# Routing of a mixture-of-experts layer in three batches, with token lists in DRAM and one expert tile ahead of the table

## The reference

```python
# 1: windowed attention with sinks -> x (3072, 512)
# 2: dense stage
h = x @ w_in                      # 512 -> 2048
x = (h * np.cos(h)) @ w_out       # 2048 -> 512
# 3: top-1 mixture of 8 experts
logits = x @ w_gate + modality_bias[modality_id]
e_idx = np.argmax(logits, axis=1)
probs = softmax(logits);  gate_w = probs[np.arange(N), e_idx]
for e in range(8):
    mask = e_idx == e
    h = np.maximum(x[mask] @ w1[e], 0.0)          # 512 -> 1024
    out[mask] = gate_w[mask, None] * (h @ w2[e])  # 1024 -> 512
```

## Time and profile before

| | us |
|---|---|
| median of 3 runs | 1177.29 (1176.71 to 1179.24) |
| profiled execution, its time | 1176.95 |
| profiled execution, its span | 1175.1 |
| PE busy in the span | 1118.3 (95%) |
| DVE busy | 720.3 (61%) |
| ACT busy | 482.8 (41%) |
| POOL busy | 87.6 (7%) |

### The profile page before, as it was taken

How to read it: one execution, slowest core, us unless ns; L and a number is a source line. 1 busy time by engine, 2 the same in 40 slices (tenths; PEclk the granted TensorE clock), 3 DMA queues, 4 the chain that set the end, 5 groups by cost and what they waited for, 6 DMA issues and landing times.

```text
span 1175.1 us, 20461 instructions
## 1 busy us (share of the span) xinstructions
PE 1118.3 (95%) x6348; PEld 935.4 (80%) x6349; DVE 720.3 (61%) x1849; ACT 482.8 (41%) x1079; POOL 87.6 (7%) x174
## 2 busy tenths in 40 slices
PE   6999999989999999999999999996799999999996
PEld 5777777767888888888888888885689999899895
DVE  7889888865458757757757757766663222342221
ACT  5777777754333333333333334332452211331221
POOL 0000000010000000000000000000121221221121
PEclk9999999999999999999999999997699999999998
DMA  5554544432002001002002000002672110131110
GB/s 121 147 146 145 145 132 135 138 116 87 1 1 72 1 1 71 0 0 72 0 0 72 0 0 36 1 1 106 202 235 68 54 54 19 40 120 38 36 53 17
DMA packets 34140, 78.72 MB, mean 67 GB/s; under 512 B 10414, under 2 KB 10414, under 8 KB 33968
## 3 DMA queue, kind: packets, MB, share of 16 engines
q1 hardware_dynamic: 29456, 65.60, 17.9%
q0 software_dynamic: 4640, 12.59, 3.2%
HBM read 60.87 MB, written 19.92 MB: 69 GB/s over the span
## 4 chain that ended last, share of the span: by engine, by line
PE 86%; DMA 3%; DVE 3%; SPq 3%; issue 3%; ACT 1%; POOL 0%; DVEq 0%; POOLq 0%; ACTq 0%
PE bank L1359 23%; PE bank L1373 23%; PE bank L1478 14%; PE bank L1466 12%; PE bank L1234 5%; DMA v_sink<-v_n 3%; PE bank L1268 3%; PE bank L1279 2%; PE bank L1246 2%; PE bank L1448 1%; SPq L405 1%; SPq L397 1%; PE bank L1439 1%; PE bank L1236 1%; SPq L400 0%
## 5 line engine op out<-in xcount | busy, mean ns | idle before, releaser
L1359 PE MATMUL bank<-x_hi,w_hi 128*128 128x512 f32 x384 | 152.4, 397 | 4.8 <-issue 4.1
L1194 DVE SCALAR_TENSOR_TENSOR h_lo<-bank,h_hi 128x256 fp32r<-128x256 f32 x112 | 47.5, 424 | 173.6 <-ACT h_hi L756 173.3
L1373 PE MATMUL bank<-w_hi,g_hi 128*128 128x512 f32 x384 | 152.3, 397 | 0.5 <-DVE g_lo L1009 0.5
L1359 PE MATMUL bank<-x_hi,w_lo 128*128 128x512 f32 x384 | 152.7, 398 | 0.0
L1359 PE MATMUL bank<-x_lo,w_hi 128*128 128x512 f32 x384 | 152.6, 397 | 0.0
L1373 PE MATMUL bank<-w_hi,g_lo 128*128 128x512 f32 x384 | 152.0, 396 | 0.0
L1373 PE MATMUL bank<-w_lo,g_hi 128*128 128x512 f32 x384 | 151.8, 395 | 0.0
L1478 PE MATMUL bank<-xg_hi,w_hi 128*128 128x256 f32 x448 | 127.4, 284 | 4.3 <-DVE xg_lo L1188 2.7
L1234 PE MATMUL bank<-k_sb,qz 128*128 128x256 f32 (+1 forms) x384 | 115.0, 401 | 17.2 <-DMA v_sink<-v_n 17.1
L1478 PE MATMUL bank<-xg_hi,w_lo 128*128 128x256 f32 x448 | 127.9, 285 | 0.0
L1478 PE MATMUL bank<-xg_lo,w_hi 128*128 128x256 f32 x448 | 127.5, 285 | 0.0
(11 more groups left out here) (164 smaller groups left out, 2083.4 us busy)
## 6 DMA issues: line engine op xcount, KB each, us to landing
raw<-w_expert SPq DMA_DIRECT2D x32, 512.0 KB, 4.4
raw<-w_dense SPq DMA_DIRECT2D x16, 512.0 KB, 4.6
k_sb<-k_t SPq DMA_DIRECT2D x16, 384.0 KB, 3.4
qz<-q_t SPq DMA_DIRECT2D x32, 192.0 KB, 4.1
v_sb<-v_n SPq DMA_DIRECT2D x16, 384.0 KB, 4.3
xT_scratch<-x_stage SPq DMA_DIRECT2D x16, 384.0 KB, 4.6
x_raw<-xT_scratch SPq DMA_DIRECT2D x6, 1024.0 KB, 5.4
y_scratch<-y_sb SPq DMA_DIRECT2D x6, 1024.0 KB, 4.3
```

The costliest lines, as they stand in the source:

```text
L1194: dve.scalar_tensor_tensor(out=h_lo[f % 4][:, :], in0=EH_BANK[f % 2][:, 0:TT], scalar=0.0, in1=h_hi[f % 4][:, :].bitcast(F32), op0=ALU.max ...
L1359: last = pe.matmul(H_BANK[f % 2][:, :], a[:, w], b[:, k, :], start=x == 0, stop=x == 3 * KD - 1)
L1373: last = pe.matmul(Y_BANK[t][:, :], a[f % 4][:, t * P:(t + 1) * P], b[:, w], start=f == 0 and x == 0, stop=f == FB1 - 1 and x == 2)
```

## The change

Tokens are routed in three batches (tiles of 128 tokens): 16, then 4, then the last 4. Routing of a batch is now: DVE makes `onehot` and a running sum `seen`; PE makes ranks (`ranks`, two or three matmuls); DVE makes a row number `slot_i = expert * 3072 + rank` and the gate, and POOL scatters (token, gate) pairs of 8 bytes into `list_scratch` in DRAM (`list_tokens`, one indirect transfer for 128 tokens). No selection matrices and no `slot_ids` remain. The list is first filled with 8192, which is out of bounds for the gathers and scatters. Batch 0 is routed in chunks 4 and 5 of the dense stage, batch 1 in the last blocks of chunk 5, batch 2 inside the first expert tile.

After batch 0 `choose_first_expert` takes the expert with most tokens among the first 2048. Its weights are loaded after the last early logit, its first tile is gathered and transposed in chunk 5 (block 11), and `expert_hidden(0, ...)` stands right behind the dense stage on PE. The other experts follow in the order of their counts (`plan_tiles`, `fill_table`).

In POOL's loop each tile's list entries are now loaded from DRAM (`load_entries`), taken into `next_ids` and `next_gates`, and held in `now_ids` and `now_gates` for the scatter. `g_hi` and `g_lo` have three buffers where they had four. The chunks of the dense stage are written out on PE and ACT too. Exponentials of the gates are computed in three batches on ACT.

```diff
+        BATCHES = ((0, 16, 192), (16, 4, None), (20, 4, 64))
@@ sync
+            sp.wait_ge(early_logits, CT * NE * (NCH - 1))
+            sp.wait_ge(first_expert_made, 1)
+            e0 = sp.value_load(first_expert[0:1, 0:1], min_val=0, max_val=NE - 1)
+            for f in range(5):
+                load_piece_of(e0, 0, f)
             store_chunk(NCH - 1)
+            for f in range(5, EP):
+                load_piece_of(e0, 0, f)
             sp.wait_ge(table_made, 1)
@@ gpsimd
+            def list_tokens(batch):
+                t0, nt, _ = BATCHES[batch]
+                pool.wait_ge(slots_made, batch + 1)
+                for t in range(t0, t0 + nt):
+                    pool.indirect_dma_start(
+                        out=list_dram[:, :], out_offset=bass.IndirectOffsetOnAxis(ap=slot_i[:, t:t + 1], axis=0),
+                        in_=entry[:, t, :], in_offset=None,
+                        bounds_check=NE * N - 1, oob_is_err=False).then_inc(listed, 16)
+            def load_entries(row):
+                pool.dma_start(landed[:, :, :], list_dram[bass.ds(row, TT), :].rearrange("(j p) w -> p j w", p=P)).then_inc(entries_loaded, 16)
...
+            list_tokens(0)
+            pool.wait_ge(listed, 16 * BATCHES[1][0])
+            pool.wait_ge(first_expert_made, 1)
+            first_row = pool.value_load(first_expert[0:1, 1:2], min_val=0, max_val=NE * N - N)
+            load_entries(first_row)
+            take_entries(0)
+            pool.wait_ge(y_stored, 16 * (NCH - 2))
+            pool.wait_ge(x_lo_made, KD * NCH)
+            hold_entries()
+            gather(0, tokens=BATCHES[1][0] * P)
+            list_tokens(1)
+            list_tokens(2)
+            pool.wait_ge(listed, 16 * NT)
...
+            pool.wait_ge(tile_rows_made, 1)
+            pool.wait_ge(table_made, 1)
...
             with pool.Fori(0, n_tiles) as t:
+                row = pool.value_load(tile_row[0:1, bass.ds(t + 1, 1)], min_val=0, max_val=NE * N - TT)
+                load_entries(row)
+                take_entries(t + 1)
                 pool.wait_ge(xg_turned, 2 * t + 2)
                 pool.wait_ge(gathered, 32 * t + 32)
                 gather(t + 1)
-                pool.tensor_copy(scatter_ids[:, :], slot_ids[:, bass.ds(2 * t, 2)]).then_inc(scatter_ids_made, 1)
...
+                hold_entries()
@@ vector, dense(c)
+                    if c == NCH - 2 and f == FB1 - 2:
+                        count_seen(0)
+                    if c == NCH - 1 and f == 2:
+                        make_slots(0)
+                        make_gates(0)
+                    if c == NCH - 1 and f == 3:
+                        choose_first_expert()
+                    if c == NCH - 1 and f == FB1 - 4:
+                        split_rows(0, FIRST_TURN)
+                        add_bias(1, logits[:, 16:20, :])
+                        find_top(1)
+                        choose(1)
+                    if c == NCH - 1 and f == FB1 - 3:
+                        count_seen(1)
+                    if c == NCH - 1 and f == FB1 - 2:
+                        make_slots(1)
+                        make_gates(1)
@@ tensor
+                    if c == NCH - 1 and f == 1:
+                        ranks(0, RANKS)
+                    if c == NCH - 1 and f == FB1 - 5:
+                        turn_rows(0, FIRST_TURN)
+                    if c == NCH - 1 and f == FB1 - 2:
+                        ranks(1, RANKS)
...
-                pe.matmul(bank[1][:, 0:NE * NT], ones[:, :], by_tile, start=True, stop=True).then_inc(counts_done, 1)
+            turn_rows(1, ET_BANK)
+            expert_down(0, FB2 - 1, 0, 0)
```

More of the change, by code:

```diff
@@ L214, in build_program @@
-        xg = x_raw[:, 0:2, :]
+            gate = top
+        yT_last = [late[:, t, :] for t in range(CT)]
+        y_out = [late[:, CT + j, :] for j in range(2)]
+        h_hi = [g_hi[i // 2][:, TT * (i % 2):TT * (i % 2 + 1)] for i in range(4)]
+        h_lo = [g_lo[i // 2][:, TT * (i % 2):TT * (i % 2 + 1)] for i in range(4)]
+        gate_rows = raw[:, :, :].rearrange("p a b -> p (a b)").rearrange("p (e d) -> p e d", e=NE)
+        empty_list = y_sb[:, 0, 0:2 * NE * NT].rearrange("p (n w) -> p n w", w=2)
@@ L1061, in _ @@
             dve.wait_ge(iota_made, 12)
[L1062 to L1063 removed]
+            n = link(dve.tensor_scalar(lower[:, :, :], lower[:, :, :], 0.0, None, ALU.is_lt))
             after(n)
@@ new lines, in _ @@
+            keep_rest(0, 5)
+            fill_table()
+            split_expert(0, 7, 0)
+            for f in range(6, FB2):
+                keep_rest(0, f)
+            end_tile(0)
+            dve.wait_ge(table_made, 1)
+            last = dve.value_load(table[0:1, T_END:T_END + 1], min_val=1, max_val=MAXT)
+            with dve.If(last > 1):
+                expert_tile(1, split=(1, 1))
+                with dve.If(last > 2):
+                    with dve.Fori(2, last) as t:
+                        expert_tile(t)
@@ L1390, in dense, with ranks, turn_rows @@
                     hidden(c + 1, 0)
-            dense(0)
-            with pe.Fori(1, NCH - 1) as c:
-                dense(c)
+            def ranks(batch, to):
+                t0, nt, counts = BATCHES[batch]
+                pe.wait_ge(onehot_made, batch + 1)
+                pe.matmul(to[:, 0:nt * NE], before[:, :], onehot[:, t0:t0 + nt, :].rearrange("p t e -> p (t e)"), start=True, stop=False)
+                last = pe.matmul(to[:, 0:nt * NE], ones[:, :], seen[:, t0:t0 + nt, :].rearrange("p t e -> p (t e)"), start=False, stop=True)
+                if counts is not None:
+                    last = pe.matmul(to[:, counts:counts + NE], ones[:, :], seen[:, t0 + nt, :], start=True, stop=True)
+                last.then_inc(ranks_done, 1)
+            def turn_rows(t, banks):
+                pe.wait_ge(gathered, 32 * t + 32)
+                for j in range(2):
+                    for k in range(KD):
+                        last = pe.transpose(banks[j][:, k * P:(k + 1) * P], xg[:, j, k * P:(k + 1) * P], ident[:, :])
+                    last.then_inc(xg_turned, 1)
             LAST = NCH - 1
-            dense(LAST, last_chunk=True)
+            for c in range(NCH):
+                dense(c, last_chunk=c == LAST)
             def last_down(f, t):
```

749 lines of the change are left out of this document (417 added, 332 removed).

## The result

The changed kernel takes 1182.79 us (median of 20 runs, 1179.16 to 1186.93) where the kernel before takes 1177.30 (20 runs, 1176.30 to 1179.24). The ratio is 1.0050, 95% interval 1.0041 to 1.0058: slower by 0.5%. Two later measurements gave 1.0043 (1.0030 to 1.0056) and 1.0023 (1.0012 to 1.0034). The forecast was 1165.5 us, range 1156 to 1178. The profiled execution took 1182.92 us, with a span of 1181.3; the prediction's sum for a profiled execution was 1165.1.

A forecast was written before the change was run, and what follows sets the result against it. PE's work was taken to bound the expert stage, with serial routing ahead of tile 0 as the one hole. 1176.95 - 12.4 (PE ends earlier) + 0.6 (end) = 1165.1, so 1165.5 as median; range 1156 to 1178 us.

The forecast's parts named there:

- The dense stage ends 2.9 us later.: Dense stage: added ranks and transposes cost PE 2.0 us, and DVE's added operations 0.9.
- gaps from written-out code: Dense stage: gaps of DVE or PE from code now written out, listed as a sign of being wrong, without a size.
- Two register loads ... landing 2.3: 838.8.: POOL, table at 828.5 to tile 1's rows: register loads 0.9, entries 1.0 + 2.4, copies and wait 1.4, then gathers, landing at 838.8.
- The issue of `load_entries` 1.0 ..., landing 2.4 after that.: POOL's loading of list entries: 1.0 us to issue and 2.4 to land, as for the scatter.
- my 16.4 us: Routing ahead of tile 1: logits done at 812.1, table at 828.5, before the dense stage's 2.9 us.
- A full tile still hides it, by 2.0.: POOL's loop in full tiles: rows land 17.9 us into the tile and are needed at 19.9, so no stall.
- A change of expert costs 1.4 us more.: Expert stage behind tile 1's start: one more change of expert, +1.4 us.
- a cold start: Tile 1's first 36 passes run at the lower clock level after the stall, +2.6 us.
- At the end ... +0.6.: Behind PE's last product: the last tile splits a dummy expert's weights and two copies follow the scatter, +0.6 us.
- POOL's loop becomes the bound: Rival, expert tiles: entries land after 6.8 us instead of 2.4, each full tile's rows 2.4 late, near 1205; chance 0.12.
- The first gather is late: Rival, chunk 5: scatters cost 2.6 us instead of 1.31, PE stalls 11 us, 1176.5 in all; chance 0.07.
- My chance of 0.14 for slower: Whole kernel: chance 0.14 of slower, against faster 0.82 and same 0.04.

The follow-up runs named there:

- b_tail: Kernel before, with expert loops of PE, ACT and DVE cut to four experts and a POOL drain each round between gathers and scatter: 1172.70 us, ratio 0.9969.
- b_lists: Kernel before, plus sixteen POOL scatters of 128 pairs of 8 bytes in chunk 5, with made-up values nobody reads: 1178.52 us, ratio 1.0014.
- a_cut: Changed kernel, with expert loops on PE, ACT and DVE cut to the three experts that have tokens: 1177.79 us, ratio 1.0004.
- a_again: Changed kernel run once more without any edit: 1183.09 us.
- a_drain: a_cut plus a POOL drain at the end of each round of its loop: 1177.72 us, ratio 1.0012.
- a_third: Changed kernel run a third time without any edit: 1180.29 us, ratio 1.0023.
- a_terms: Changed kernel with four edits together, those of a_pieces, a_quiet and a_cut, and POOL drains behind the gathers: 1165.87 us, ratio 0.9903.
- a_early: Changed kernel, with tile 1's entries loaded and rows gathered in chunk 5, ahead of batch 1 and 2 scatters and the table: 1161.04 us, ratio 0.9850.
- a_prefetch: a_early, with list entries of tile t+2 loaded between the gathers of t+1 and the scatter of t: 1156.58 us, ratio 0.9826.
- a_pieces: Changed kernel, with the first expert's weight pieces 5 to 7 issued without waiting for chunk 5's store to land: 1178.09 us, ratio 1.0007.
- best1: a_prefetch and a_pieces together, plus POOL drains behind gathers from tile 1 on and PE's expert loop ended by the count in use: 1142.37 us, ratio 0.9724.
- a_quiet: Changed kernel, with the second expert's weights held back until the rows of tile 1 have landed: 1179.12 us, ratio 1.0011.
- a_order: Changed kernel, with an expert of exactly one token placed second instead of last: 1182.74 us, ratio 1.0044.
- a_pace: Changed kernel, with each of batch 0's sixteen scatters waiting for one more early logit: 1186.31 us, ratio 1.0070.
- b_flat: Kernel before, with chunks 1 to 4 of the dense stage written out on PE and ACT instead of looped: 1177.40 us, ratio 1.0001.

## Why the prediction was wrong

The profiled execution is 17.8 us above the sum. By its own steps:

1. *The start.* +1.0. At the start of the dense stage PE's clock was at its lower level for longer than before (mean 0.83 between 255 and 275 us, before 0.91). Nothing in the change touches that place, and it is spread: the second hidden group starts 1.1 us sooner than before in b_tail, 0.5 later in b_lists and 3.4 later in a_cut.

2. *"The dense stage ends 2.9 us later."* It ended 8.0 later, 1.0 of them from the start. The terms that I had sized held: 0.88 us for the ranks of batch 0, 0.87 for the eight transposes, 0.38 for the ranks of batch 1, and DVE some 0. The other 4.8 are the pause in blocks 7 and 8 of chunk 5. I had named gaps from written-out code as a sign, but given them no price. The pause was 1.4 to 1.6 us in the four profiles from a_again to a_drain, which were taken together, and absent in the other nine of kernels with the change. So it explains this profile, and only part of the median: in a_third it was absent, and the median was 1180.29.

3. *"Two register loads ... landing 2.3: 838.8."* POOL's path from the table to the rows of tile 1 is the step that failed most clearly: 10.3 us in the sum, 16.5 measured (837.1 to 853.6). The sum lets POOL start at the table and puts the list scatters of batch 2 at nothing, though POOL waits for them first. The last one landed at 839.6, 2.5 us behind the table: 6.7 us from its issue, where a scatter of 2 KB rows takes 2.8 (median of the kernel before), and I had priced lists by such a scatter. Then the register loads took 2.3 for 0.9, `load_entries` 5.3 for 3.4, the copies 1.7 for 1.4. The two gathers took 4.8 for 4.7, as predicted.

   The landing of the list scatters is not contention with the weights. While the last one was under way the DMA engines had a share of 0.04 (0.01 in a_terms, where it took 6.76 us), and the second expert's pieces were issued from 838.7 on. Those of batch 0, at a share of 0.02, landed 4.9 to 5.9 us behind their issue in a_early, a_prefetch, a_pieces, a_terms and best1. The Trainium skill (DMA: Bandwidth & Descriptors, Specifications) says that transfers under 512 bytes are read, modified and written. That alone does not give these times: the scatters of b_lists write runs of 8 bytes too, at the same place of the program, and land in 3.5. All 24 of a_early and the 16 of b_lists:

```profile
DMA to landing us min/median/max: 4.0/5.2/8.8
```

```profile
DMA to landing us min/median/max: 3.3/3.5/3.8
```

   In b_lists the rows of one scatter are consecutive and lie in one of two small tensors, in the change they are spread over the experts' lists in a larger one. No run tests what makes the difference.

4. *"The issue of `load_entries` 1.0 ..., landing 2.4 after that."* In most tiles it is 2.2 from the start of the issue, better than the 3.4, but it was 5.3 in tile 0 and 3.2 in tile 1, beside the next weights. a_quiet shows the cause: without the weights it lands in 2.2 in tile 0. I had priced this transfer by a transfer of a quiet stretch. From the logits to the table my 16.4 us met 18.1. The steps up to the logits took 1.1 us less than I had, and those from the rows to tile 1 2.0 less (4.1 for 6.1). Together 6.2 + 1.7 - 1.1 - 2.0 = 4.8.

5. *"A full tile still hides it, by 2.0."* Not in tile 1, where the scatter took 5.6 us, the entries 3.2 and the gathers 4.9: `turn_rows(2)` waited 3.2 us, and with the clock's fall tile 1 lasted 28.45 us, +4.9. The other full tiles gave back 0.13 each, the half tile at 6 was late by 1.95 where I had 2.2.

6. *"A change of expert costs 1.4 us more."* The one behind tile 6 cost no more than that. The last one cost 3.8 us and then 2.4 for the lower clock. a_order shows that the cost goes with the one-token expert and not with the end. On the other side, tile 1 itself ran at the upper level where I had put 2.6 us for a cold start. Steps 5 and 6 together: the stretch behind tile 1's start is 4.8 longer than predicted.

7. *"At the end ... +0.6."* It was +3.7. I took the stretch behind PE's last product as fixed. It is two queues side by side: PE reads the table entries of empty experts, 2.76 us each, and POOL drains. Ordering by count puts all empty experts last, and the added transfers lengthen the drain. a_cut shows that ending PE's loops alone gives 0.9 us, and a_drain and b_tail what both together are worth.

1.0 + 4.1 + 4.8 + 4.8 + 3.1 = 17.8, the end counted here without the 0.6 that I had. The terms come from one profile of the changed kernel, and the pause and the slow branch differ from one profile to the next. a_terms takes out the end, the weights beside the entries and the wait for the store ahead of piece 5, and the kernel takes 1165.9 us. That shows that these waits are worth 14.4 us together; that the result is the forecast's number is luck. PE's last product ends at 1156.5, 5.0 us later than I had forecast, and the stretch behind it takes 7.9 us in place of the 13.6 of the forecast, by edits that shorten it in the kernel before too.

Of the rivals, "POOL's loop becomes the bound" was wrong for the steady state, as argued, and its mechanism was right in the first tile behind the table. "The first gather is late" was wrong: the gathers were issued at 762.8, and PE came at 780.1, 4.7 of it by the pause; a_pace issued them 11.5 us later and made PE wait 3.2. A scatter took 1.33 us from issue to issue, as I took it (1.31). My chance of 0.14 for slower put most of it on a mechanism that acts in every tile. What made the kernel slower were places that act once.

The cause of the pause in chunk 5 is likely late code, and why the code is late stays open. Blocks of 16 KB of code come every 30 us there (b_flat has them where the kernel before, with its loop, has none, so they are PE's). Counted from the start of the hidden group of block 6, the next block landed after 11.9 to 12.4 us in the nine profiles without a pause and in b_lists, after 16.2 to 16.7 in the four with 1.4 to 1.6 us of it, and after 18.0 in the first, with 4.8. Beside the scatters such a block took 2.1 to 3.1 us in place of about 1, but it did so in profiles without a pause too, b_lists among them; a late start of the fetch goes with the pause, and no run shows what starts it late. a_pace could not show more, since its partner had no pause either.

The branch at the last change of expert took 0.33 us in three profiles of fourteen (a_again, a_third, best1) and 3.3 to 3.5 in the ten others that have it there. In these three, and in none of the ten, one more block of 16 KB had been fetched some 20 us behind the start of tile 7, long before the branch; a_order, where the slow branch stands elsewhere, is left out. In a_again that block started at 1023.5, and the changed kernel's first profile has none between 1003.1 and 1139.7. What makes the fetch come early in some executions is open.

## What to carry to other kernels

Price a small transfer by what else moves in that stretch, and one that writes 8-byte runs to DRAM not by one that writes rows: from issue to landing, 2.2 us became 5.3 beside weights, and a list scatter took 5.2 (median of a_early) and at its worst place 6.7, where rows take 2.8. When work is moved into a hole, list what the next stage still waits for: tile 1 needed none of the routing that it waited for, and loading it early was worth some 19 to 22 us (a_early against three medians of the changed kernel), more than the 11.8 that I had forecast for the whole change. Read the end of the program like any other stage, register loops and drains included; it gave some 4 us in the kernel before for two edits.

## What the runs showed of the hardware

- POOL's drain at the end of the program grows by 0.082 us for each transfer that POOL has issued: 4.80 us with 58 transfers, 6.11 with 74, 8.07 with 98. Only those since its last drain count: it takes 0.2 us where the loop drains behind the gathers and three or four transfers follow (b_tail, best1, a_terms). The drains inside the loop cost more than that rule gives: 0.77 us (median) for the five transfers of a round in a_drain, where all have landed, and 3.2 to 8.4 in the tiles behind the gathers in b_tail, best1 and a_terms, where they have just been issued. There POOL waits for the tile's results anyway, and the time fell.
- A taken branch of PE can cost 3.3 us. In the changed kernel it started at 1138.7, and a 16 KB block of PE's code was fetched at 1139.7. The Trainium skill (Runtime: NRT & Kernel Launch, Instruction fetch mechanics) says that a branch out of the blocks at hand waits for a fetch; the traces agree, with 0.33 us where one more block had come before. It also prefers code that is written out, and there b_flat shows neither gain nor loss (ratio 1.0001).
- Reading three entries of a table and branching costs PE's queue 2.76 us an expert, and this goes on behind its last matmul.
